# Attention stage unrolled, V's chunks made one stream by quarter of w1 and w2 with seven held for the last batch, smaller pieces in the first loads, state rows stored batch by batch

## The reference

```python
scores  = scale * x @ state^T;  a  = exp(scores - rowmax);   a  /= a.sum(-1) + 1e-9
scores2 = scale * state @ x^T;  a2 = exp(scores2 - rowmax);  a2 /= a2.sum(-1) + 1e-9
x = concatenate([a @ state, a2 @ x], axis=2)      # per batch 512 + 32 rows
x = ((x @ w1) * (x @ w2)) @ w3 @ w_out            # first layer,  512 -> 1024 -> 512
h = x @ w_in;  out = (h - tanh(h)) @ w_out        # second layer, 512 -> 2048 -> 512
```

## Time and profile before

| what | us |
| --- | --- |
| median of 3 runs | 1359.01 |
| lowest and highest | 1358.49, 1360.21 |
| the profiled execution, time | 1360.77 |
| the profiled execution, span | 1359.0 |

### The profile page before, as it was taken

One profiled execution on the slowest core, in us unless ns is written; L12 is line 12 of the kernel. 1 busy time (PEld: TensorE's weight loads), 2 busy tenths in 40 slices (PEclk: granted clock), 3 DMA queues, 4 the chain that ended last, 5 costly groups with the idle time before them and its releaser, 6 DMA issues. The chain is left out here.

```text
span 1359.0 us, 17300 instructions
## 1 busy us (share of the span) xinstructions
PE 1322.4 (97%) x6272; PEld 1101.6 (81%) x6272; DVE 818.7 (60%) x1342; ACT 578.5 (43%) x1073; POOL 16.0 (1%) x14
## 2 busy tenths in 40 slices
PE   5999899999999999999999999999999999999996
PEld 5889788888888888878888888887888888888885
DVE  3777443444445443367867667666676676776764
ACT  4555332433434433244544444444444344443443
POOL 0111000000000000000000000000000000000000
PEclk9999799999999999999999999999999999999999
DMA  8789112322233321221110100100101001010000
GB/s 355 248 266 319 49 66 90 93 78 90 70 112 101 100 93 29 71 77 48 47 47 16 47 1 16 47 8 10 47 16 47 1 15 47 12 35 7 8 32 16
DMA packets 57654, 97.82 MB, mean 72 GB/s; under 512 B 3960, under 2 KB 37752, under 8 KB 53368
## 3 DMA queue, kind: packets, MB, share of 16 engines
q1 hardware_dynamic: 53384, 86.52, 19.5%
q10 hardware_dynamic: 4208, 10.49, 2.2%
HBM read 62.39 MB, written 34.60 MB: 71 GB/s over the span
## 5 line engine op out<-in xcount | busy, mean ns | idle before, releaser
L1213 ACT ACTIVATE hq<-bank 128x512 f32<-128x512 f32 (+1 forms) x144 | 83.0, 576 | 412.9 <-PE bank L1316 412.8
L1316 PE MATMUL bank<-ysp_hi,wi_hi 128*128 128x512 f32 (+1 forms) x576 | 221.6, 385 | 2.0 <-issue 1.3
L1270 DVE TENSOR_TENSOR hw<-hw,hq 128x512 f32<-128x512 f32 (+1 forms) x144 | 95.4, 663 | 212.0 <-ACT hw L1218 212.0
L1316 PE MATMUL bank<-ysp_hi,wi_lo 128*128 128x512 f32 (+1 forms) x576 | 220.6, 383 | 0.0
L1316 PE MATMUL bank<-ysp_lo,wi_hi 128*128 128x512 f32 (+1 forms) x576 | 220.2, 382 | 0.0
L1338 PE MATMUL wide<-wz_hi,gsp_hi 128*128 128x512 f32 x544 | 213.4, 392 | 3.6 <-DVE gsp_lo L1264 2.5
L1338 PE MATMUL wide<-wz_lo,gsp_hi 128*128 128x512 f32 x544 | 212.3, 390 | 0.0
L1338 PE MATMUL wide<-wz_hi,gsp_lo 128*128 128x512 f32 x544 | 212.0, 390 | 0.0
L1316 PEld LDWEIGHTS bank<-ysp_hi,wi_hi 128*128 128x128 f32 x576 | 108.0, 188 | 25.0 <-issue 1.7
L1316 PEld LDWEIGHTS bank<-ysp_hi,wi_lo 128*128 128x128 f32 x576 | 108.7, 189 | 24.0
L1316 PEld LDWEIGHTS bank<-ysp_lo,wi_hi 128*128 128x128 f32 x576 | 108.2, 188 | 23.8
(11 more groups left out here) (121 smaller groups left out, 1988.5 us busy)
## 6 DMA issues: line engine op xcount, KB each, us to landing
v_dram<-vs SPq DMA_DIRECT2D x64, 256.0 KB, 4.1
vr<-v_dram SPq DMA_DIRECT2D x64, 256.0 KB, 2.9
xT<-in_x_cols SPq DMA_DIRECT2D x8, 1024.0 KB, 7.8
y_dram<-ysb SPq DMA_DIRECT2D x8, 1024.0 KB, 4.5
yr<-y_dram SPq DMA_DIRECT2D x32, 256.0 KB, 3.6
out<-ysb SPq DMA_DIRECT2D x8, 1024.0 KB
xs<-in_x_rows SPq DMA_DIRECT2D x7, 1024.0 KB, 6.9
wraw<-in_moe_w_in ACTq DMA_DIRECT2D x16, 256.0 KB, 3.1
```

The lines of the kernel that those rows point to most:

```text
L1213: act.activation(hq[:, f % 2, 0:w], ph[f % 2][:, 0:w], ACT.Square).then_inc(sq_done, 1)
L1270: dve.tensor_tensor(u, u, q, ALU.mult).then_inc(w2_done, 1)
L1316: mm = pe.matmul(ph[f % 2][:, 0:w], wi[s][:, c, f * P:(f + 1) * P], ysp[k][u][c][:, 0:w], start=c + m == 0, stop=c == KC - 1 and m == LAST)
```

## The change

- The attention stage is written out for all 8 entries; no loop is left on SP, ACT, DVE and PE (POOL keeps its loop).
- V's chunks are numbered 0 to 63 in one stream: chunk v has q = v // 16, i = v // 4 % 4, c = v % 4. So q goes slowest, and each quarter of w1 and w2 is needed 16 chunks after the one before. Entry 0 makes 8 chunks, entries 1 to 7 make 7 each (four before `a_turn`, one between `a_turn` and `scores_turn`, two after), and the last 7 (57 to 63) stand behind entry 7 among the last batch's own steps.
- w quarter 0 is loaded by ACT right behind the first piece of sT; quarter 1 by SP behind xT of entries 0 and 1 and xs of entry 0; quarters 2 and 3 in entries 1 and 3. They are loaded to the place of the low part (`w_raw` has the address of `w12_lo`) and split there. ACT and DVE split quarter 0 ahead of everything of entry 0, the others in entries 1, 3 and 5.
- sT is loaded in four pieces of 256 KB by pair of batches, and is split in groups of two pairs of batches of one q, one group an entry.
- On DVE `rows_invert` and the split of `sT` move behind `tokens_scale`. Entry 7's exponential of `a` (ACT), row sums and inversion (DVE) move behind its `a2` work.
- At the end, SP stores the state rows by batch: 8 DMAs of 32 rows (64 KB), the first four after the first copy, the others after the second.
- `base` and `end` are rounded to 128 bytes.

```diff
-        base = (nc.sbuf_usable_end - nc.sbuf_bytes_remaining + 63) // 64 * 64
-        end = nc.sbuf_usable_end // 32 * 32
+        base = (nc.sbuf_usable_end - nc.sbuf_bytes_remaining + 127) // 128 * 128
+        end = nc.sbuf_usable_end // 128 * 128
...
+    FIRST = [0] + [7 * e + 1 for e in range(1, B + 1)] + [CHUNKS]
+    def of_chunk(v):
+        return v // 16, v // 4 % 4, v % 4
...
# SP
+        load_xT(sp, 0)
+        load_sT(sp, 1)
+        load_xT(sp, 1)
+        load_xs(sp, 0)
+        load_w(sp, 1)
+        load_xs(sp, 1)
+        stored = 0
+        for e in range(B):
+            if e + 2 < B:
+                load_xT(sp, e + 2)
+            if e in (1, 3):
+                load_w(sp, (e + 3) // 2)
+            while 2 * stored + 1 < FIRST[e] + 4:
+                store_v(stored)
+                stored += 1
+            if 2 <= e + 1 < B:
+                load_xs(sp, e + 1)
...
# ACT
+        load_sT(act, 0)
+        load_w(act, 0)
+        load_sT(act, 2)
+        load_sT(act, 3)
...
+        def entry(e):
+            v = FIRST[e]
+            if e == 0:
+                split_s(0)
+                split_w(0)
+            act.wait_ge(scored, e + 1)
...
+            chunk(v)
+            if e == 0:
+                chunk(v + 1)
+            else:
+                turn_a2_half(e - 1)
+            chunk(v + 2)
+            if e == 0:
+                chunk(v + 3)
+            if e in (1, 3, 5):
+                split_w((e + 1) // 2)
+            if e > 0:
+                turn_a_half(e - 1)
+            chunk(v + 4)
+            if e + 1 < B:
+                split_s(e + 1)
+            if e + 1 < B:
+                exp_a(e)
+            chunk(v + 5)
+            exp_a2(e)
+            chunk(v + 6)
+            if e == 0:
+                chunk(v + 7)
+        for e in range(B):
+            entry(e)
+            if e == B - 3:
+                prefetch(act)
+        exp_a(B - 1)
+        v = FIRST[B]
+        chunk(v + 1)
+        chunk(v + 3)
         turn_a2_half(B - 1)
+        chunk(v + 4)
+        chunk(v + 6)
...
# DVE
+            rows_max(e)
+            if e > 0:
+                chunk(v + 1)
+                turn_a2_half(e - 1)
+                chunk(v + 3)
+            if e in (1, 3, 5):
+                split_w((e + 1) // 2)
+            if e > 0:
+                sread(e - 1)
+                turn_a_half(e - 1)
+            rows_sub(e)
+            tokens_max(e)
+            if e + 1 < B:
+                rows_sum(e)
+            tokens_scale(e)
+            if e + 1 < B:
+                rows_invert(e)
+                split_s(e + 1)
+        v = FIRST[B]
+        chunk(v)
+        rows_sum(B - 1)
+        rows_invert(B - 1)
+        chunk(v + 2)
         turn_a2_half(B - 1)
+        chunk(v + 5)
         sread(B - 1)
...
# PE, behind entry 7
+        v = FIRST[B]
+        for n in range(4):
+            chunk(v + n)
+        a2_turn(B - 1)
+        chunk(v + 4)
+        chunk(v + 5)
+        sread(B - 1)
+        a_turn(B - 1)
+        chunk(v + 6)
...
# SP, end of stage_moe2
-        sp.wait_ge(o_copied, J * B + NSTATE // P)
         each = P // NS
-        for k in range(NSTATE // P):
-            sp.dma_start(out_v[k * each:(k + 1) * each, S:ROWS, :], ob[:, k, :]).then_inc(o_out, 16)
-        sp.wait_ge(o_out, 16 * (B + NSTATE // P))
+        for b in range(B):
+            if b % each == 0:
+                sp.wait_ge(o_copied, J * B + b // each + 1)
+            at = b % each * NS
+            sp.dma_start(out_v[b, S:ROWS, :], ob[at:at + NS, b // each, :]).then_inc(o_out, 16)
+        sp.wait_ge(o_out, 16 * 2 * B)
```

More of the change, by code:

```diff
@@ L376, in gpsimd @@
+        while stored < CHUNKS // 2:
+            store_v(stored)
+            stored += 1
+        for m in range(RING // 2):
+            sp.wait_ge(v_out[m], 32 * CHUNKS // RING)
     def gpsimd(pool):
@@ L451, in entry @@
-            if not last:
-                split_s(e + 1, i + par, 1 - par)
-            if not first(e):
-                if isinstance(e, int) and e == 1:
-                    split_w(3)
-                    act.wait_ge(w_lo, 2 * KC)
-                turn_a_half(e - 1)
-            chunk(e, next(v))
-            chunk(e, next(v))
-            exp_a(e)
-            act.wait_ge(tok_bias, e + 1)
-            if not first(e):
-                for k in range(2):
-                    act.wait_ge(turned[k], turn_a2(e - 1) + 1)
@@ L467, in entry @@
-            for g in range(G):
-                act.activation(a2[:, g, :], px[:, g * W:(g + 1) * W], ACT.Exp, scale=SCALE, bias=tbias[:, g:g + 1],
-                               accum_out=tsum[:, g:g + 1]).then_inc(tok_exp, 1)
-            if first(e):
-                split_w(2)
-            for n in v:
-                chunk(e, n)
-        def pair(i, last=False):
-            entry(i, 0)
-            entry(i, 1, last)
-        pair(0)
-        with act.Fori(1, PAIRS - 1) as i:
-            pair(i)
@@ L736, in pair @@
-        def pair(i):
-            entry(i, 0)
-            entry(i, 1)
-        pair(0)
-        with pe.Fori(1, PAIRS) as i:
-            pair(i)
+            for n in range(v + 5, FIRST[e + 1]):
+                chunk(n)
+        for e in range(B):
+            entry(e)
+        v = FIRST[B]
+        for n in range(4):
+            chunk(v + n)
         a2_turn(B - 1)
-        sread(PAIRS - 1, 1)
+        chunk(v + 4)
+        chunk(v + 5)
+        sread(B - 1)
         a_turn(B - 1)
+        chunk(v + 6)
```

237 lines of the change are left out of this document (86 added, 151 removed).

## The result

The changed kernel takes 1327.63 us (median of 4 runs, 1325.81 to 1329.06) where the kernel before takes 1358.75 on the same chip (4 runs, 1357.36 to 1360.21): a ratio of 0.9769, 95% interval 0.9757 to 0.9781. The forecast was 1347.3 with a range of 1342.0 to 1353.5. It is 31.1 us faster, not 11.7, and the time lies outside the range. The profiled execution took 1327.2, with a span of 1324.7 against 1359.0.

A forecast was written before the change was run, and what follows sets the result against it. PE was taken as busy for 97% of the span, so only the first 158 us and the very end could give time back. 1.7 + 6.8 - 1.3 + 1.0 + 3.5 = 11.7 us, from 1359.0 to 1347.3, range 1342 to 1353.5.

The forecast's parts named there:

- At nothing. The alignment of `end`: Tiles at the top of SBUF move by 96 bytes: copies there and to `aT` take the same time, so no gain.
- Term 3: Attention loop: period 15.7 us, PE waiting about 1.1 us per entry for DVE's copy of a chunk; a loss of 1.3 us.
- It is wrong if the period is 14.9: Sign against the forecast: a `scores_turn` period of 14.9 us, where 15.7 was expected.
- Term 4: Tail of the last batch: waits of 1.8 and 2.1 us, one slow-clock spell losing 2.0; a gain of 1.0 us.
- Terms 1 and 2: Start, up to the end of `a_turn(0)`: xT lands earlier, 1.7 us; waits for sT and w and a slow spell go, 6.8.
- The DMAs of entries 1 and 3: Stores of chunks 4 and 18 behind xT and w barely land in time; a miss costs about 1 us each.
- Term 5: End of the kernel: state rows stored in eight DMAs over 16 engines, 0.5 us an issue; a gain of 3.5 us.
- Rival (a): The loop isn't held by DVE, or the tail keeps its clock: 1342 us; chance 0.15.
- (b): The clock stays low through the tail's sread: 1353 us; chance 0.11.
- (f): Start: w quarter 0 isn't there at the end of the first scores, so 3.7 us stay: 1351 us; no separate chance.
- (d): Stores late in the ring of `vs` or w late: each entry some 1 us more, 1354 us; chance 0.06.
- (e): New 1.2 us waits in every entry drop the clock; at both sread and scores in six entries, 1368 us; chance 0.07.

The follow-up runs named there:

- experiment 2: The changed kernel with only the two roundings of `base` and `end` set back to 64 and 32 bytes: 1339.61 us, ratio 0.9862.
- experiment 1: The kernel before with only `base` and `end` rounded to 128 bytes: 1345.75 us, ratio 0.9912.
- Experiment 6: The changed kernel with a scratch product added on POOL beside DVE's scale of `a2` in each entry: 1332.72 us, ratio 0.9801.
- experiment 8: The changed kernel with ACT's last-batch list reordered: chunk 56 copied ahead of the `a2` exponentials, chunk 63 behind the srT splits: 1326.12 us, ratio 0.9749.
- experiment 7: The changed kernel with eight chunks in every entry and none held for the tail; entry 7's `a` steps stand inside the entry again: 1341.6 us, ratio 0.9853.
- experiment 5: The changed kernel with `rows_invert` ahead of `tokens_scale` again in entries 0 to 6: 1329.82 us. Also the kernel before with POOL waiting for the `a2` scale: 1355.26 us.
- experiment 3: The kernel before with only the state rows stored batch by batch: 1354.27 us, ratio 0.9964.
- experiment 4: The changed kernel with tiles moved: `a2` alone 96 bytes off, 1326.55 us; `wi` alone 96 off, 1336.25 us; all of the top 64 off, 1338.93 us.

## Why the prediction was wrong, by its steps

**The step that failed first: "At nothing. The alignment of `end`".** It read: copies to the top and to `aT` take the same time now. That looked at who writes the tiles. The 1536 matmuls that have `wi` as their stationary operand were not looked at. The groups of the profile had the hint: layer 3's matmuls at 398, 396 and 395 ns, and others of the same form (128x512, no wait before them) at 389. The prediction should have asked why one form has two durations, and put a bound on it: 1536 matmuls at 9 ns at most is 14 us, more than its whole sum. Measured: 12.0 and 12.7 (experiments 2 and 1). A forecast that carries this term at its measured size says 1335.

**Term 3, the loop (forecast -1.3).** The scale was taken at 2.41 us from the earlier trace rows, as a property of the instruction. It depends on a neighbour: the change puts the inversion, which releases POOL, behind the scale, and the scale falls to 0.88. The prediction even moved the inversion in its list, and charged it 0.5, without asking whom it releases. The period is 14.87 where 15.7 was forecast; DVE waits for ACT now, and PE in the entries no more for DVE. "It is wrong if the period is 14.9" is the sentence that came true. Experiment 6 puts the slow scale back and finds 5.1 us and a period of 15.40, so 0.5 of the 0.8 an entry is the scale, and 0.3 is the chain itself, which was taken as too long.

The traces fit a rule here. The Trainium skill ("SBUF — State Buffer", Who interferes with whom) says that a `tensor_scalar` of DVE in its two-port mode and an instruction of GpSimd hold a shared pair of ports exclusively, the first one for its whole length. By that rule, as an estimate, the first scale ends when the product has ended and its own 0.49 us of work is done, and the second takes its 0.48. The trace of the kernel before agrees in the main: the product ends at 52.40, the first scale takes 2.02 us and ends at 52.68, the second takes 0.47. No row names the mode in which the scale runs.

**Term 4, the tail (forecast +1.0).** Chunk 58 waits 1.31 (forecast 1.8), chunk 59 waits 0.47 (2.1, behind the scale again), s1 waits 1.45 behind chunk 63's copy (the prediction had 1.55 between the end of chunk 63 and s1). There is no spell at the lower clock (1.00 granted from 128 to 146; with the second wait at 1.80 and 2.29 in experiments 6 and 8 there is one), and s1 starts at 143.28 with sread, a_turn and s1 at full speed. What the held chunks do for the clock was right: experiment 7 without them has the 7.06 us sread back. Too much in the term were the spell (2.0) and 1.6 of the second wait.

**Terms 1 and 2, the start (forecast 1.7 + 6.8).** Right in what happens; together they came to 10.0, not 8.5. xT landed for a start at 7.02 (forecast 7.0), the first chunk stands right behind, at 13.84, neither w quarter is waited for, and no second slow spell follows. `a_turn(0)` ended at 34.74, where 36.2 was forecast. 0.6 of it at least is that the chunks' matmuls reached the length of the upper clock 4.0 us after the first of them (13.84 to 17.82), where the prediction kept twelve matmuls at half speed. The rest lies in the waits of chunk 7 (0.17, forecast 0.5) and chunk 8 (none, forecast 0.8).

**The DMAs of entries 1 and 3.** "That covers them barely; a miss costs about 1 us each." One of the two missed: PE waited 1.43 at 68.49, and the entry took 16.59 us where the others take 14.87. The chain, in the timelines of SP and then of ACT of the kernel after:

```profile
56.43 0.33 SPq L330 DMA_DIRECT2D xT<-in_x_cols  x1
56.80 0.91 SPq L339 DMA_DIRECT2D w_raw<-in_moe_w  x2
57.81 6.89 SPq L352 DMA_DIRECT2D v_dram<-vs  x8
```

```profile
67.84 0.60 ACT L418 ACTIVATE vs<-bank 128x512 f32<-128x512 f32 x1 [2.84 <-DMA v_dram<-vs]
```

The stores stand behind xT and w in SP's queue, ACT waits 2.84 us for a slot of `vs`, and PE for ACT. This is the thin place of the kernel after: the same miss cost 4.1 us in the profile of experiment 5 and 8.1 in that of experiment 7, where the clock fell behind it.

**Term 5, the end (forecast 3.5).** 4.2 alone (experiment 3), 4 in the trace. An issue is 0.455 us, not 0.5, and 4.9 us from the last copy to the end, not 5.5. The share of the DMA engines is 0.5, not near 1. The forecast counted on 16 engines for the new DMAs; a share of 0.5 neither shows nor excludes that.

**The account.** From 1347.3 to 1327.6 are 19.7 us: 12.0 the tiles' place (experiment 2), 5.1 the scale (experiment 6), 0.7 the end (experiment 3), and 1.9 that remain. Each comes from runs whose 95% interval reaches some 2 us to either side, so the 1.9 may be nothing. In the trace, s1 starts 8.4 ahead of the forecast 151.7: 1.5 up to `a_turn(0)`, 5.0 in six periods, 0.4 for the wait of entry 2 that didn't come, 3.4 in the tail (t + 17.5 in place of t + 20.9), less the 1.7 of entry 3. The scale has its share in the periods and the tail; which part of the rest goes to what wasn't measured apart. Rival (a), 1342, had the loop and the tail right and missed the place of the tiles as well; experiment 2, which is the change without that place, stands at 1339.61. Of the rivals (b) to (f) only (d) came about, in one entry. The clock didn't drop in the loop of the kernel after, but (e) named a danger that is real: in experiments 5 and 7 it did drop in entry 3, ahead of the scores. The sum in (e) is wrong by its own terms: 3.5 us at both sread and scores in six entries are 42, not 21.

## What to carry to other kernels

When one form of instruction has two durations in the groups of a profile (398 and 389 ns of a matmul, 1246 and 484 ns of a scale), find out what sets them apart before using either in a sum: here it was where the stationary operand stands, and who works beside it. An edit is "at nothing" only after every group that reads or writes the moved tiles has been looked at, the longest stage first; 2 to 3% on 1536 instructions outweighs every wait that was removed. And when an instruction is moved, ask whom it releases as well as what it costs in its queue.

## What the runs showed of the hardware that wasn't expected

- With the tiles at the top of the map 96 bytes off a multiple of 128, the matmuls of layer 3 (128x512) take 3% longer (0.234 against 0.227 us from start to start; 12 to 12.7 us of 1359), with no wait between them. 8.6 of this are the stationary operand `wi` alone. All of the top 64 off is about as bad as 96 (11.3, experiment 4). In the stage of `w3T` 96 off costs 6 ns of the mean if only the stationary operand is off, and nothing if both are; in layer 3 both off still cost most of it.
- Two fp32 scales of 128x512 on DVE take 0.88 us alone and 2.2 to 2.4 beside a product of 1.9 us on POOL.
- Eight DMAs of 64 KB are issued in 3.64 us, 0.455 each, and keep the DMA engines half busy; two of 256 KB took 1.34 us to issue and had a share of 0.27.
- The length of a wait alone doesn't tell whether TensorE's clock falls behind it. The granted clock stayed at 1.00 behind waits of 1.43 us (entry 3 of the kernel after), of 1.83 (the same place in experiment 2) and of 1.31 and 0.47 (the tail of the kernel after). It fell behind one of 1.23 (experiment 5), behind 1.75 and 0.78 (experiment 7), and in the tail behind 1.31 and 1.80 (experiment 6).
